# Attention, router and two feed-forward blocks on one core: even and odd heads given one layout of V, and the exponentials of the attention moved one step earlier on ScalarE

## The chip, the core and the metric

The kernel runs on one core of one Trainium2 chip. The core has TensorE (PE in the rows, with its weight loads as PEld), VectorE (DVE), ScalarE (ACT), GpSimd (POOL) and SyncE (SP, which only issues DMAs here). Each of them works through its own list of instructions in order; they meet through semaphores. PSUM is the memory that TensorE writes its results to, SBUF the working memory, and 16 DMA engines move data between SBUF and HBM. The metric is the time of one execution on the device in microseconds (us).

## What is computed

The inputs are q, k and v of 4 batches, 8 heads, 768 positions and 64 dimensions, and the weights of a router and of two feed-forward blocks. In short:

```python
scores = q @ k.T / 8                     # per batch and head, 768 x 768
keep = (key < 4) | (0 <= query - key < 128)
a = softmax(where(keep, scores, -1e9))
x = (a @ v), heads side by side          # 3072 rows x 512
logits = x @ w_gate + modality_bias[modality_id]
e = argmax(logits); p = softmax(logits)[e]
x2 = p * (relu(x @ w1[e]) @ w2[e])       # 8 experts
h = x2 @ w_in
out = (h * sigmoid(1.702 * h)) @ w_out
```

A query thus sees the first 4 positions (the sinks) and the last 128. Everything is float32. Many products are made from values that are split in a rounded and a remaining part.

## The kernel before

The attention comes first and takes about the first fifth of the time; the router, the experts and the last block follow it. The change touches the attention alone.

**Tiles and steps.** A head's 768 queries are 6 tiles of 128. A batch has 8 heads x 6 tiles = 48 tiles, and tile n of a batch is tile i = n mod 6 of head h = n div 6. All engines walk through the same numbered steps (`each_step`), and in step n each does its part for tiles of different age:

- TensorE: `scores` of tile n (L610, L611), in every second head a piece of `weigh_gates` in the head's second and third step (L667, L671), `turn_probs` of tile n-3 (transposes, L622, and for a head's last tile the sinks too, L626), and `weigh_values` of tile n-4 (L647, for the last tile of a head also L652).
- VectorE: `mask_scores` of tile n (L1090: adds the mask and takes the row's maximum, in two instructions), `move_gates` in one step of each pair of heads, `move_probs` for a head's last tile only (L1101, L1102), and in a head's fifth step `finish_head` of the head before (L1107 to L1116: row sums, reciprocals, scaled results). At the end of a batch it also sums the router's logits (L1152).
- ScalarE: `move_probs` of tile n-3 for the other five tiles of a head (L879, transposed probabilities from PSUM to SBUF), then `exps` of tile n-1 (L854), then, in the first step of a head, `pack_sinks` of the head before (L860), and `spread_sinks` once in each pair of heads (L869).
- GpSimd: `split_qk`, which splits q and k of a head in two parts, up to four heads ahead (L531 to L540).
- SyncE: the loads of q and k (L336), of V (L341 and, for the four sink rows, L343), of V transposed (L352), the stores of finished pairs of heads (L364), and pieces of w_in (L359).

**What waits for what.** Within an engine the order is the order written in its `step`. `exps` of a tile waits for that tile's mask, `turn_probs` of a tile for its `exps`, `move_probs` for the transposes, and `weigh_values` for `move_probs`. Where the steps of two batches meet, `each_step` does the new batch's step first.

**The layout of V.** Each pair of heads has for each block of keys one row of 146 words in `v_sb`: 73 for the even head and 73 for the odd one. A head's 73 are its 64 values, a one (its product is the row's sum of probabilities) and 8 router logits of the key. The even head has the order logits, one, values, the odd head values, one, logits, so that the values of both are 128 neighbouring words, which one DMA row of 512 bytes fills. `OWN`, `DEN` and `LOG` give where values, one and logits lie in each. `v_sinks` has the same layout for the four sink keys. Where the ones go, and the logits, VectorE writes with one instruction for each half of a pair.

Of the kernel before, what the change touches and what calls it, by code (L numbers as in the profile page):

```python
# [22 lines left out]
P = 128  # L23
# [4 lines left out]
ALU = mybir.AluOpType  # L28
# [12 lines left out]
def program(nc, qkT, vT, vP, modality, w_gate, bias, w1, w2, w_in, w_out, out, n_sink, window):  # L41
    B, H, D, _, S = qkT.shape
    DM = H * D
    E, _, F = w1.shape
# [40 lines left out]
    LW, VW = 64, 80  # L85
    VEXT = D + 1 + E
    OWN, DEN, LOG = (E + 1, 0), (E, D), (0, D + 1)
    VPAIR = 2 * VEXT
    COPIES = P // SINKS
# [28 lines left out]
    with ExitStack() as ctx:  # L118
# [52 lines left out]
        k_lo = place("k_lo", [P, SLOT, KEYS], F32R)  # L171
        v_sb = place("v_sb", [P, PAIRS, QT, VPAIR])
        x_sb = place("x_sb", [P, QT, DM])
# [10 lines left out]
        p_sinks = place("p_sinks", [P, P])  # L184
        v_sinks = place("v_sinks", [P, PAIRS, SINK_T, VPAIR])
        scratch = place("scratch", [P, 8])
# [144 lines left out]
        def _(sp):  # L331
# [6 lines left out]
            def load_v(b, c):  # L338

                both = slice(OWN[0], OWN[0] + P)  # L340
                sp.dma_start(v_sb[:, c, :, both], vP[b, c]).then_inc(v_loaded[c], 16)  # L341
                for t in range(SINK_T):
                    sp.dma_start(v_sinks[t * SINKS:(t + 1) * SINKS, c, t, both],  # L343
                                 vP[b, c, 0:SINKS, 0])\
                      .then_inc(v_loaded[c], 16)
# [247 lines left out]
        def _(pe):  # L593
# [35 lines left out]
            def weigh_values(b, n):  # L629
                h, i = divmod(n, QT)  # L630
                c, half = divmod(h, 2)
                if dve_takes[i]:
                    pe.wait_ge(pT_moved_dve, b * moved(True, HT) + (moved(True, n + 1) + AHEAD))
                else:
                    pe.wait_ge(pT_moved_act, b * moved(False, HT) + (moved(False, n + 1) + AHEAD))
                if i == 0:

                    pe.wait_ge(heads_done, b * H + (h - 1 + AHEAD))
                    if half == 0:
                        pe.wait_ge(v_loaded[c], b * (LOADS_V * 16) + LOADS_V * 16)  # L640
                        pe.wait_ge(vw_moved, 2 * (b * PAIRS + c + 1))
                        pe.wait_ge(sinks_marked, 2 * PAIRS + 2)
                keys = [max(i - 1, 0) + k for k in range(blocks[i])]

                o = psum[:, O_ps[h % 2], i * VW:i * VW + VEXT]
                for k, kb in enumerate(keys):
                    mm = pe.matmul(o, pT[:, n % 2, k * P:(k + 1) * P],  # L647
                                   v_sb[:, c, kb, half * VEXT:(half + 1) * VEXT],
                                   start=(i == 0 and k == 0), stop=(k == len(keys) - 1), skip_group_check=True)
                if i == QT - 1 and SINK_T:  # L650

                    mm = pe.matmul(psum[:, O_ps[h % 2], FIRST_S * VW:QT * VW]  # L652
                                   .rearrange("p (t n) -> p t n", n=VW)[:, :, 0:VEXT], pT_sinks[:],
                                   v_sinks[:, c, :, half * VEXT:(half + 1) * VEXT],
                                   start=False, stop=True, skip_group_check=True)
                mm.then_inc(pv_done, 1)

            def weigh_gates(b, c, part):

                g = b * PAIRS + c  # L660
                if part == 0:
                    pe.wait_ge(wg_loaded, 32)
                    pe.wait_ge(vt_loaded[g % 2], g // 2 * 16 + 16)
                    if g:
                        pe.wait_ge(vw_moved, 2 * g)
                for t in range(part * HALF_T, (part + 1) * HALF_T):
# [172 lines left out]
        def _(act):  # L839
# [169 lines left out]
        def _(dve):  # L1009
# [12 lines left out]
            dve.memset(wg_sb[:], 0.0).then_inc(cleared, 1)  # L1022
            for half in range(2):
                at = half * VEXT + DEN[half]
                dve.memset(v_sb[:, :, :, at:at + 1].rearrange("p c t o -> p (c t) o"), 1.0).then_inc(sinks_marked, 1)
            for s in (logits_out, xsT_split, y_moved, x2T_split, o_moved_dve):
# [77 lines left out]
            def finish_head(b, h):  # L1104
                dve.wait_ge(pv_done, b * HT + ((h + 1) * QT + AHEAD))
                heads = psum[:, O_ps[h % 2], 0:QT * VW].rearrange("p (t d) -> p t d", t=QT)
                dve.tensor_scalar(rden[:, 0, :], heads[:, :, DEN[h % 2]], 1e-9, None, ALU.add).then_inc(dve_step, 1)  # L1107
# [4 lines left out]
                dve.tensor_tensor(lg_parts[:, h, :].rearrange("p (t e) -> p t e", t=QT), heads[:, :, LOG[h % 2]:LOG[h % 2] + E],  # L1112
                                  per_row.broadcast_to([P, QT, E]), ALU.mult).then_inc(part_added, 1)
                if h % 2 == 0:
                    dve.wait_ge(x_stored[h // 2], b * 16 + DMA)
                dve.tensor_tensor(x_sb[:, :, h * D:(h + 1) * D], heads[:, :, OWN[h % 2]:OWN[h % 2] + D],  # L1116
                                  per_row.broadcast_to([P, QT, D]), ALU.mult).then_inc(heads_done, 1)

            def move_gates(b, c):
# [5 lines left out]
                for half in range(2):  # L1125
                    at = half * VEXT + LOG[half]
                    dve.tensor_tensor(v_sinks[0:rows, c, :, at:at + E],
                                      row[:, :, half * E:(half + 1) * E].broadcast_to([rows, SINK_T, E]),
                                      sink_pick[0:rows].rearrange("p (t o) -> p t o", o=1)
                                      .broadcast_to([rows, SINK_T, E]),  # L1130
                                      ALU.mult)
                for half in range(2):
                    at = half * VEXT + LOG[half]
# [279 lines left out]
```

## Time and profile before

| | |
|---|---|
| median of 3 runs | 1169.98 us (1169.49 to 1170.28) |
| the profiled execution, its own time | 1169.98 us |
| its span, first to last instruction | 1167.9 us |
| mean granted TensorE clock | 0.970 of full speed |
| TensorE busy (matmuls) | 1108.2 us, 95% |
| TensorE weight loads | 937.1 us, 80% |
| VectorE, ScalarE, GpSimd busy | 427.7, 376.6, 273.2 us |

TensorE is busy nearly everywhere. The chain that ended last, which is followed back from the last instruction through what released each step, consists of TensorE's work to 93%. A change elsewhere moves the end only where it makes TensorE wait, or ends a wait of TensorE. A matmul's end is modelled in this profile, so a short wait is seen better in the row of the weight load than in that of the matmul.

### The profile page before, as it was taken

The page shows a single profiled execution, that of the slowest core. Times are in us where ns is not written, and L with a number is a line of the kernel's source. Part 1 is how long each engine was busy: PE and PEld are TensorE (multiplying, and loading weights), DVE is VectorE, ACT ScalarE, POOL GpSimd, SP SyncE. Part 2 cuts the span into 40 slices and gives each one's busy share as a digit, 9 for nine tenths or more (in the row PEclk, how much of TensorE's full clock was granted, in tenths as well). Part 3 has the DMA queues.
Part 4 walks back from the last instruction along what each step waited for, and adds up shares of the span by engine and source line. Part 5 has one row for each costly group of instructions (what it writes and reads, how often), then busy time and mean ns, then how long its engine had stood idle before and what let it go on. Part 6 is the DMA issues. An engine that isn't in the chain of part 4 may idle for free.

```text
span 1167.9 us, 18474 instructions
## 1 busy us (share of the span) xinstructions
PE 1108.2 (95%) x5844; PEld 937.1 (80%) x5845; DVE 427.7 (37%) x1098; ACT 376.6 (32%) x779; POOL 273.2 (23%) x327
## 2 busy tenths in 40 slices
PE   9999999925999999999959999999999999999998
PEld 9999999824888888888847888888888888888886
DVE  5665666684222233212335223223322322222222
ACT  3666666512222133222325222222222222222221
POOL 8898888002751112112110000000000000000000
PEclk9999999956999999999988999999999999999999
DMA  9999997145111124111051002002001000100000
GB/s 218 244 256 233 232 229 190 47 154 184 45 44 37 45 79 150 40 45 45 27 190 54 1 1 72 0 0 72 0 0 56 16 0 27 45 0 0 36 1 36
DMA packets 58669, 91.98 MB, mean 79 GB/s; under 512 B 7936, under 2 KB 32768, under 8 KB 58624
## 3 DMA queue, kind: packets, MB, share of 16 engines
q1 hardware_dynamic: 54464, 77.79, 24.2%
q0 software_dynamic: 4160, 13.63, 3.5%
q8 instruction: 23, 0.38, 0.1%
q14 instruction: 22, 0.18, 0.1%
HBM read 72.01 MB, written 19.40 MB: 78 GB/s over the span
## 4 chain that ended last, share of the span: by engine, by line
PE 93%; DVE 3%; issue 1%; DMA 1%; ACT 1%; DVEq 0%; ACTq 0%; POOLq 0%; POOL 0%; SPq 0%
PE psum L799 8%; PE psum L800 8%; PE psum L801 8%; PE psum L816 8%; PE psum L817 8%; PE psum L818 7%; PE psum L647 6%; PE psum L731 4%; PE psum L733 4%; PE psum L732 4%; PE psum L756 4%; PE psum L758 4%; PE psum L757 4%; PE psum L622 3%; PE psum L610 2%; PE psum L743 2%
## 5 line engine op out<-in xcount | busy, mean ns | idle before, releaser
L1357 DVE TENSOR_TENSOR g<-psum,g 128x512 f32<-128x512 f32 x96 | 66.4, 691 | 312.0 <-ACT g L978 312.0
L978 ACT ACTIVATE g<-psum 128x512 f32<-128x512 f32 x96 | 57.3, 597 | 320.2 <-PE psum L801 320.1
L799 PE MATMUL psum<-x2T,win_hi 128*128 (+1 forms) x384 | 152.9, 398 | 1.4 <-DVE x2T L1349 1.4
L800 PE MATMUL psum<-x2T,win_hi 128*128 (+1 forms) x384 | 152.4, 397 | 0.0
L816 PE MATMUL psum<-w_hi,gT_hi 128*128 128x512 f32 x384 | 152.4, 397 | 0.0
L801 PE MATMUL psum<-x2T,win_lo 128*128 (+1 forms) x384 | 152.3, 397 | 0.0
L817 PE MATMUL psum<-w_lo,gT_hi 128*128 128x512 f32 x384 | 150.4, 392 | 0.0
L818 PE MATMUL psum<-w_hi,gT_lo 128*128 128x512 f32 x384 | 149.7, 390 | 0.0
L647 PE MATMUL psum<-v_sb,pT 128*128 128x73 f32 x704 | 105.9, 269 | 1.8 <-DVE pT L1102 0.3
L1090 DVE CUSTOM_DVE_ANT_0 s_msk<-psum,mask_sb 128x260 f32<-128x260 f32 (+1 forms) x192 | 74.9, 404 | 74.8 <-PE psum L611 39.7
L647 PEld LDWEIGHTS psum<-v_sb,pT 128*128 128x128 f32 x704 | 93.4, 191 | 8.3 <-DVE pT L1102 5.6
L854 ACT ACTIVATE probs<-s_msk,negmax 128x260 f32<-128x260 f32 (+1 forms) x192 | 93.4, 495 | 12.4 <-DVE negmax L1090 12.2
L1360 DVE TENSOR_TENSOR gT_lo<-g,gT_hi 128x512 fp32r<-128x512 f32 x96 | 66.5, 692 | 65.9 <-ACT gT_hi L982 65.9
L756 PE MATMUL psum<-w_hi,hT_hi 128*128 128x512 f32 x208 | 83.9, 403 | 5.8 <-DVE w_lo L1288 5.8
L799 PEld LDWEIGHTS psum<-x2T,win_hi 128*128 128x128 f32 x384 | 72.4, 189 | 18.8 <-DVE x2T L1349 1.8
L731 PE MATMUL psum<-w_hi,xsT_hi 128*128 128x512 f32 x208 | 84.6, 407 | 2.3 <-DVE xsT_lo L1303 2.3
L801 PEld LDWEIGHTS psum<-x2T,win_lo 128*128 128x128 f32 x384 | 72.4, 189 | 17.8
L800 PEld LDWEIGHTS psum<-x2T,win_hi 128*128 128x128 f32 x384 | 72.6, 189 | 16.9
L818 PEld LDWEIGHTS psum<-w_hi,gT_lo 128*128 128x128 f32 x384 | 72.1, 188 | 16.3
L816 PEld LDWEIGHTS psum<-w_hi,gT_hi 128*128 128x128 f32 x384 | 72.1, 188 | 15.8
L817 PEld LDWEIGHTS psum<-w_lo,gT_hi 128*128 128x128 f32 x384 | 72.2, 188 | 15.2
L982 ACT CAST gT_hi<-g 128x512 fp32r<-128x512 f32 x96 | 59.5, 620 | 75.6 <-DVE g L1357 75.6
(184 smaller groups left out, 1863.1 us busy)
## 6 DMA issues: line engine op xcount, KB each, us to landing
qk_raw<-qkT SPq DMA_DIRECT2D x64, 384.0 KB, 7.8
stage<-w SPq DMA_DIRECT2D x12, 1024.0 KB, 6.5
vT_sb<-vT SPq DMA_DIRECT2D x16, 384.0 KB, 7.4
v_sb<-vP SPq DMA_DIRECT2D x16, 384.0 KB
x_rows<-x_sb SPq DMA_DIRECT2D x16, 384.0 KB, 3.4
x<-y_rows SPq DMA_DIRECT2D x24, 256.0 KB, 3.2
out<-o_out SPq DMA_DIRECT2D x24, 256.0 KB, 2.1
win_raw<-w_in SPq DMA_DIRECT2D x16, 256.0 KB, 8.6
```

Of the source, the lines that this page charges most:

```text
L647: mm = pe.matmul(o, pT[:, n % 2, k * P:(k + 1) * P], v_sb[:, c, kb, half * VEXT:(half + 1) * VEXT], start=(i == 0 and k == 0), stop=(k == ...
L731: pe.matmul(psum[:, HB[hf], :], xsT_hi[:, c, :], hi, start=(c == 0), stop=False)
L756: pe.matmul(psum[:, YB, :], hT_hi[:, f, :], hi, start=(f == 0), stop=False)
L799: pe.matmul(bank, wh, hi, start=(c == 0), stop=False)
L800: pe.matmul(bank, wh, lo, start=False, stop=False)
L801: mm = pe.matmul(bank, win_lo[:, c, f * P:(f + 1) * P], hi, start=False, stop=(c == CH - 1))
L816: pe.matmul(psum[:, OB[t], :], gh, hi, start=(f == 0), stop=False)
L817: pe.matmul(psum[:, OB[t], :], gh, lo, start=False, stop=False)
L818: mm = pe.matmul(psum[:, OB[t], :], gT_lo[:, f % 4, t * P:(t + 1) * P], hi, start=False, stop=(f == F2C - 1))
L854: act.activation(probs[:, n % RING, 0:width[i]], s_msk[:, n % RING, 0:width[i]], ACT.Exp, bias=negmax[:, n % 8:n % 8 + 1], scale=-1.0).the ...
L1090: dve.tensor_tensor_reduce(s_msk[:, n % RING, 0:width[i]], psum[:, S_ps[n % 3], 0:width[i]], mask_sb[:, min(i, MASKS - 1), 0:width[i]], -S ...
L1360: dve.tensor_tensor(gT_lo[:, f % 4, :], g32[:, f % 2, :], gT_hi[:, f % 4, :].bitcast(F32), ALU.subtract).then_inc(gT_split, 1)
```

## The change

It has two parts.

**One layout for both heads of a pair.** `v_sb` and `v_sinks` get for each head a row of 80 words: 64 values, the one, 8 logits and 7 unused. The two constants `DEN`, `LOG` are the same for both heads, and `OWN` is gone. The load of V now writes 64 neighbouring words (256 bytes) at a time where it wrote 128. VectorE fills the ones and the logits of both halves with one instruction; `vw_moved` and `sinks_marked` are counted accordingly.

**ScalarE's order.** In step n it does `exps` of tile n, no longer of tile n-1, and `pack_sinks` stands ahead of it.

```diff
-    VEXT = D + 1 + E
-    OWN, DEN, LOG = (E + 1, 0), (E, D), (0, D + 1)
-    VPAIR = 2 * VEXT
+    DEN, LOG, VEXT = D, D + 1, D + 1 + E
...
-        v_sb = place("v_sb", [P, PAIRS, QT, VPAIR])
+        v_sb = place("v_sb", [P, PAIRS, QT, 2, VW])
...
-                both = slice(OWN[0], OWN[0] + P)
-                sp.dma_start(v_sb[:, c, :, both], vP[b, c]).then_inc(v_loaded[c], 16)
+                sp.dma_start(v_sb[:, c, :, :, 0:D].rearrange("p t h d -> p (t h) d"),
+                             vP[b, c].rearrange("p t h d -> p (t h) d")).then_inc(v_loaded[c], 16)
                 for t in range(SINK_T):
-                    sp.dma_start(v_sinks[t * SINKS:(t + 1) * SINKS, c, t, both],
+                    sp.dma_start(v_sinks[t * SINKS:(t + 1) * SINKS, c, t, :, 0:D],
                                  vP[b, c, 0:SINKS, 0])\
...
-                                   v_sb[:, c, kb, half * VEXT:(half + 1) * VEXT],
+                                   v_sb[:, c, kb, half, 0:VEXT],
...
             def step(b, n):
                 if TURN_LAG <= n < HT + TURN_LAG:
                     move_probs(b, n - TURN_LAG)
-                if 1 <= n <= HT:
-                    exps(b, n - 1)
                 if n % QT == 0 and n and n <= HT and SINK_T:
                     pack_sinks(b, n // QT - 1)
+                if n < HT:
+                    exps(b, n)
                 if n < HT and n % (2 * QT) == VW_AT:
                     spread_sinks(b, n // (2 * QT))
...
             for c in range(PAIRS):
-                for half in range(2):
-                    dve.tensor_copy(v_sinks[:, c, :, half * VEXT + DEN[half]], sink_pick[:]).then_inc(sinks_marked, 1)
+                dve.tensor_copy(v_sinks[:, c, :, :, DEN],
+                                sink_pick[:].rearrange("p (t o) -> p t o", o=1).broadcast_to([P, SINK_T, 2]))\
+                   .then_inc(sinks_marked, 1)
...
-                for half in range(2):
-                    at = half * VEXT + LOG[half]
-                    dve.tensor_copy(v_sb[:, c, :, at:at + E],
-                                    psum[:, VW_ps, 0:QT * LW].rearrange("p (t n) -> p t n", n=LW)
-                                    [:, :, half * E:(half + 1) * E]).then_inc(vw_moved, 1)
+                dve.tensor_copy(v_sb[:, c, :, :, LOG:VEXT],
+                                psum[:, VW_ps, 0:QT * LW].rearrange("p (t n) -> p t n", n=LW)[:, :, 0:2 * E]
+                                .rearrange("p t (h e) -> p t h e", h=2)).then_inc(vw_moved, 1)
```

How ScalarE's order moves is seen best where one head ends and the next begins. These are its instructions before, in the first batch from tile 15 of head 2 on. An exponential has `probs` as its result, a move has `pT`, packing has `p_sinks`; the shape 128x128 marks a head's first tile. In order they are: exponential 15, move 14, exponential 16, move 15, exponential 17, packing, move 16, exponentials 18 and 19, move 18.

```order
L854 ACTIVATE probs<-s_msk,negmax 128x260
L879 COPY pT<-psum 128x256
L854 ACTIVATE probs<-s_msk,negmax 128x260
L879 COPY pT<-psum 128x256
L854 ACTIVATE probs<-s_msk,negmax 128x260
L860 COPY p_sinks<-probs 128x16
L879 COPY pT<-psum 128x256
L854 ACTIVATE probs<-s_msk,negmax 128x128
L854 ACTIVATE probs<-s_msk,negmax 128x260
L879 COPY pT<-psum 128x128
```

Now ScalarE has the same stretch as follows (the lines have moved up by two). In order: exponential 16, move 14, exponential 17, move 15, packing, exponential 18, move 16, exponentials 19 and 20, move 18.

```order
L852 ACTIVATE probs<-s_msk,negmax 128x260
L877 COPY pT<-psum 128x256
L852 ACTIVATE probs<-s_msk,negmax 128x260
L877 COPY pT<-psum 128x256
L858 COPY p_sinks<-probs 128x16
L852 ACTIVATE probs<-s_msk,negmax 128x128
L877 COPY pT<-psum 128x256
L852 ACTIVATE probs<-s_msk,negmax 128x260 x2
L877 COPY pT<-psum 128x128
```

Moves and packing keep their order among themselves; each exponential has moved ahead of one move. Exponential 17 now stands ahead of move 15, where it stood behind it.

## Rows read from the trace of the kernel before

**Rows 1.** Busy time by stage: us, busy by engine (instructions), PEclk, DMA share, GB/s.
```profile
80.00:200.00 120.00, 118.98 (x979) 112.87 (x979) 73.06 (x357) 75.81 (x222) 102.86 (x110) 1.00 0.93 230
```
**Rows 2.** Waits, 0 to 230 us: who waited for whom, us, times, longest us.
```profile
DVE s_msk L1090 <- ACT probs L854: 34.4, 54, 1.1
PEld psum L647 <- DVE pT L1102: 5.4, 17, 0.5
```
**Rows 3.** Timeline: start, us, engine, line, instruction; batch 2, steps 17 to 19, heads 2 and 3.
```profile
140.46 0.51 ACT L854 ACTIVATE probs<-s_msk,negmax 128x260 f32<-128x260 f32 x1
140.52 0.16 DVE L1107 TENSOR_SCALAR rden<-psum 128x6 f32<-128x6 f32 x1
140.88 0.37 ACT L879 COPY pT<-psum 128x256 f32<-128x256 f32 x1
141.53 0.42 DVE L1090 CUSTOM_DVE_ANT_0 s_msk<-psum,mask_sb 128x260 f32<-128x260 f32 x1
141.79 0.37 ACT L879 COPY pT<-psum 128x256 f32<-128x256 f32 x1
141.88 0.08 DVE L1090 DVE_READ_ACCUMULATOR2_ANT negmax<- 128x1 f32 x1
142.39 0.53 PEld L647 LDWEIGHTS psum<-v_sb,pT 128*128 128x128 f32 x4
```
**Rows 4.** Timeline, where head 1 of batch 2 ends and head 2 begins.
```profile
134.52 0.08 DVE L1090 DVE_READ_ACCUMULATOR2_ANT negmax<- 128x1 f32 x1
135.64 0.53 PEld L647 LDWEIGHTS psum<-v_sb,pT 128*128 128x128 f32 x4
...
142.98 0.80 ACT L854 ACTIVATE probs<-s_msk,negmax 128x128 f32<-128x128 f32 x2
```
**Rows 5.** Timeline, batch 2, steps 5 to 8, behind the logits' sum of batch 1.
```profile
128.90 0.52 PEld L647 LDWEIGHTS psum<-v_sb,pT 128*128 128x128 f32 x4
129.13 0.09 DVE L1090 DVE_READ_ACCUMULATOR2_ANT negmax<- 128x1 f32 x1
129.26 0.51 ACT L854 ACTIVATE probs<-s_msk,negmax 128x260 f32<-128x260 f32 x1 [0.58 <-DVE negmax L1090]
129.82 0.20 PEld L622 LDWEIGHTS psum<-ident,probs 128*128 128x128 f32 x2 [0.17 <-ACT probs L854]
```
**Rows 6.** Timeline, the last steps of the attention.
```profile
228.96 0.52 PEld L647 LDWEIGHTS psum<-v_sb,pT 128*128 128x128 f32 x4
228.97 0.51 ACT L854 ACTIVATE probs<-s_msk,negmax 128x260 f32<-128x260 f32 x1
```
**Rows 7.** Timeline: scores of batch 2's tile 19 and the mask behind them.
```profile
142.16 0.28 PE L611 MATMUL psum<-k_lo,q_st 128*128 128x260 f32 x1
142.66 0.43 DVE L1090 CUSTOM_DVE_ANT_0 s_msk<-psum,mask_sb 128x260 f32<-128x260 f32 x1 [0.49 <-ACT probs L854]
```
**Rows 8.** DMA queue: packets, MB, share of 16 engines; 102.6 to 103.6, then 29.0 to 30.5 us.
```profile
q1 hardware_dynamic: 489, 0.28, 104.1%
...
q1 hardware_dynamic: 2759, 0.04, 107.4%
```
**Rows 9.** Timeline: GpSimd's split of head 5 of batch 0, and the head's first scores.
```profile
36.82 0.82 POOL L531 CAST q_st<-qk_raw 128x768 fp32r<-128x768 f32 x1 [2.78 <-DMA qk_raw<-qkT]
42.32 0.23 POOL L540 TENSOR_TENSOR k_lo<-qk_raw,k_hi 128x24 fp32r<-128x24 f32 x1
...
46.62 0.31 PE L610 MATMUL psum<-k_hi,q_st 128*128 128x128 f32 x1
```
**Rows 10.** Waits of SyncE, 0 to 230 us.
```profile
SPq L364 <- DVE x_sb L1116: 86.9, 14, 11.7
```
**Rows 11.** Small instructions of VectorE, and TensorE's first transposes: timeline, then groups by line.
```profile
10.39 1.96 DVE L1058 COPY v_sinks<-sink_pick 128x4 f32<-128x4 f32 x8 [0.32 <-issue]
17.02 0.14 PEld L622 LDWEIGHTS psum<-ident,probs 128*128 128x128 f32 x1
...
L1134 DVE COPY v_sb<-psum 128x48 f32<-128x48 f32 x28 | 4.4, 199 | 0.0
```

More of the change, by code:

```diff
@@ L184, in program @@
         p_sinks = place("p_sinks", [P, P])
-        v_sinks = place("v_sinks", [P, PAIRS, SINK_T, VPAIR])
+        v_sinks = place("v_sinks", [P, PAIRS, SINK_T, 2, VW])
         scratch = place("scratch", [P, 8])
@@ L640, in weigh_values @@
                         pe.wait_ge(v_loaded[c], b * (LOADS_V * 16) + LOADS_V * 16)
-                        pe.wait_ge(vw_moved, 2 * (b * PAIRS + c + 1))
-                        pe.wait_ge(sinks_marked, 2 * PAIRS + 2)
+                        pe.wait_ge(vw_moved, b * PAIRS + c + 1)
+                        pe.wait_ge(sinks_marked, PAIRS + 1)
                 keys = [max(i - 1, 0) + k for k in range(blocks[i])]
@@ L653, in weigh_values @@
                                    .rearrange("p (t n) -> p t n", n=VW)[:, :, 0:VEXT], pT_sinks[:],
-                                   v_sinks[:, c, :, half * VEXT:(half + 1) * VEXT],
+                                   v_sinks[:, c, :, half, 0:VEXT],
                                    start=False, stop=True, skip_group_check=True)
@@ L664, in weigh_gates @@
                     if g:
-                        pe.wait_ge(vw_moved, 2 * g)
+                        pe.wait_ge(vw_moved, g)
                 for t in range(part * HALF_T, (part + 1) * HALF_T):
@@ L1022, in _ @@
             dve.memset(wg_sb[:], 0.0).then_inc(cleared, 1)
-            for half in range(2):
-                at = half * VEXT + DEN[half]
-                dve.memset(v_sb[:, :, :, at:at + 1].rearrange("p c t o -> p (c t) o"), 1.0).then_inc(sinks_marked, 1)
+            dve.memset(v_sb[:, :, :, :, DEN:DEN + 1].rearrange("p c t h o -> p (c t h) o"), 1.0).then_inc(sinks_marked, 1)
             for s in (logits_out, xsT_split, y_moved, x2T_split, o_moved_dve):
@@ L1106, in finish_head @@
                 heads = psum[:, O_ps[h % 2], 0:QT * VW].rearrange("p (t d) -> p t d", t=QT)
-                dve.tensor_scalar(rden[:, 0, :], heads[:, :, DEN[h % 2]], 1e-9, None, ALU.add).then_inc(dve_step, 1)
+                dve.tensor_scalar(rden[:, 0, :], heads[:, :, DEN], 1e-9, None, ALU.add).then_inc(dve_step, 1)
                 dve.wait_ge(dve_step, b * 2 * H + 2 * h + 1)
@@ L1111, in finish_head @@
                 per_row = rden[:, 1, :].rearrange("p (t o) -> p t o", o=1)
-                dve.tensor_tensor(lg_parts[:, h, :].rearrange("p (t e) -> p t e", t=QT), heads[:, :, LOG[h % 2]:LOG[h % 2] + E],
+                dve.tensor_tensor(lg_parts[:, h, :].rearrange("p (t e) -> p t e", t=QT), heads[:, :, LOG:VEXT],
                                   per_row.broadcast_to([P, QT, E]), ALU.mult).then_inc(part_added, 1)
@@ L1115, in finish_head @@
                     dve.wait_ge(x_stored[h // 2], b * 16 + DMA)
-                dve.tensor_tensor(x_sb[:, :, h * D:(h + 1) * D], heads[:, :, OWN[h % 2]:OWN[h % 2] + D],
+                dve.tensor_tensor(x_sb[:, :, h * D:(h + 1) * D], heads[:, :, 0:D],
                                   per_row.broadcast_to([P, QT, D]), ALU.mult).then_inc(heads_done, 1)
@@ L1125, in move_gates @@
                 for half in range(2):
-                    at = half * VEXT + LOG[half]
-                    dve.tensor_tensor(v_sinks[0:rows, c, :, at:at + E],
+                    dve.tensor_tensor(v_sinks[0:rows, c, :, half, LOG:VEXT],
                                       row[:, :, half * E:(half + 1) * E].broadcast_to([rows, SINK_T, E]),
@@ L1131, in move_gates @@
                                       ALU.mult)
-                for half in range(2):
-                    at = half * VEXT + LOG[half]
-                    dve.tensor_copy(v_sb[:, c, :, at:at + E],
-                                    psum[:, VW_ps, 0:QT * LW].rearrange("p (t n) -> p t n", n=LW)
-                                    [:, :, half * E:(half + 1) * E]).then_inc(vw_moved, 1)
+                dve.tensor_copy(v_sb[:, c, :, :, LOG:VEXT],
+                                psum[:, VW_ps, 0:QT * LW].rearrange("p (t n) -> p t n", n=LW)[:, :, 0:2 * E]
+                                .rearrange("p t (h e) -> p t h e", h=2)).then_inc(vw_moved, 1)
             def step(b, n):
```

## The prediction

> **What bounds the kernel now.** I read the busy times by stage first. In the middle of the attention TensorE's matmuls fill 118.98 of 120 us and its weight loads 112.87, at a granted clock of 1.00 [rows 1]. So the attention takes what TensorE takes, plus what TensorE waits. Next come the waits. TensorE's largest one is for VectorE's move of a head's last tile, 5.4 us in 17 places [rows 2]; there is hardly another. ScalarE is busy for 75.81 of the 120 us and VectorE for 73.06 [rows 1], so neither is a bound by its sum. What matters is when each of their results is late. That is read from the timeline, where one head passes into the next, since VectorE has its longest job there. In step 17 it starts `finish_head` at 140.52, behind mask 16, and is free for mask 17 at 141.53: 1.01 us in which no mask is made [rows 3]. The mask of a head's last tile is late in every head, and the question is who stands behind it.
>
> **ScalarE's order, away from batch ends.** Before, in step 18, ScalarE does move 15 first (141.79, 0.37 us) and exponential 17 behind it. The late mask, whose maximum is there at 141.88 + 0.08 = 141.96, holds nobody up. Tile 15 is in SBUF at 142.16, and TensorE loads it at 142.39, 0.23 us later, for work it is free to do then [rows 3].
>
> After, exponential 17 stands ahead of move 15. It can't start before the mask's maximum. Rows 5 show 0.04 us between the maximum (129.13 + 0.09 = 129.22) and the exponential (129.26), so it starts at 142.00. From an exponential's start to that of the move behind it I take 0.42 us, as from 140.46 to 140.88 [rows 3], though it takes 0.51: ScalarE overlaps the ends. So move 15 starts at 142.42 and ends at 142.79. I add 0.05 us for TensorE to see it, about what a semaphore took above, and TensorE loads at 142.84 in place of 142.39. It stands still for 0.45 us. TensorE is in order: scores 20 and all that follows stand behind this load, the wait isn't made up for, and VectorE and ScalarE are driven by TensorE's scores, so they shift with it. Bounds for one wait: 0.30 if the overlap is larger than that one row shows, 0.55 if there is none.
>
> This holds where an even head ends and an odd one begins. Where an odd head ends, TensorE has a piece of `weigh_gates` in front of the same load. There the maximum is out at 134.60 and the load comes only at 135.64, 1.04 us later; exponential (0.04 + 0.42), move (0.37) and 0.05 fit in 0.88 [rows 4]. No wait. The even heads with a `finish_head` in them and no batch end are heads 2, 4 and 6 in 4 batches: 12 x 0.45 = 5.4 us (3.6 to 6.6).
>
> **At batch ends.** In the first head of batches 1 to 3, VectorE has also the sum of the logits behind `finish_head`. The maximum of tile 5 comes at 129.22, the exponential starts at 129.26 already now (ScalarE waited 0.58 us for it), and now move 3 is behind it: 129.26 + 0.42 + 0.37 + 0.05 = 130.10, and TensorE loaded tile 3 at 128.90 [rows 5]. That is 1.20 us, less 0.17 us which TensorE today waits for the same exponential a bit later (the load at 129.82) and then no longer does: 1.03 us, 3 times, 3.1 us (2.4 to 3.6).
>
> Where two batches meet, `each_step` does the new batch's step first, so that in the first step exponential 0 of the new batch too is ahead of move 45. By the same kind of place [rows 4]: 134.60 + 0.04 + 0.42, a 128-wide exponential at 0.80 - 0.51 = 0.29, then 0.37 and 0.05, is 135.77 against 135.64. That is 0.13 us, 3 times, 0.4 us (0 to 0.8).
>
> At the attention's end no scores stand between the steps. Exponential 47 starts at 228.97 and is now ahead of move 45: 228.97 + 0.42 + 0.37 + 0.05 = 229.81 against TensorE's load at 228.96 [rows 6]. That is 0.85 us (0.4 to 0.9), and the router waits for this end.
>
> **What an earlier exponential gives.** Exponentials are ready one turn sooner for the transposes. TensorE's waits for them are the 0.17 us counted above. The larger wait, for VectorE's move of the last tile, stays: it hangs on mask 20 and the transposes, which follow TensorE's scores.
>
> **The layout.** TensorE's instructions keep their count and shapes. VectorE does 4 small copies fewer at the start, of the 8 that take 1.96 us, about 1 us less ahead of its first mask; but TensorE's own list reaches the first transposes at 17.02, 4.7 us after those copies end (10.39 + 1.96 = 12.35) [rows 11], so nothing comes of it. The copy of logits comes once for a pair instead of twice, at 199 ns each [rows 11], 16 x 0.2 = 3.2 us of VectorE in all if none of it is lost to the longer copy. It lies in a pair's fourth step, where VectorE has no `finish_head`, so it is worth nothing here. The larger clearing of `v_sinks` at the start lies ahead of VectorE's first wait for q and k. I cost these at 0, between -1 and 0.
>
> The load of V goes from 768 packets of 512 bytes to 1536 of 256: on each of 16 engines 96 packets instead of 48. The trace has no packet of 256 bytes. Nearly all packets of the one window are of 512 bytes: 16 x 1.0 us x 1.041 / 489 = 34 ns each. Those of the other are nearly all of 8 bytes: 16 x 1.5 x 1.074 / 2759 = 9.3 ns [rows 8]. A packet of 256 bytes lies between these ends, by a straight line at 22 ns. One load of V then takes 2.1 us of each engine instead of 1.6, +0.5 us (-0.7 to +1.6). Is it hidden? The DMA engines are 0.93 busy [rows 1], 12.5 us of each 13.49, the time of a pair of heads (the same load of a fourth tile stands at 128.90 and one pair later at 142.39 [rows 3, 5]). With 0.5 us more they still keep up. The tightest place is early: the q and k of head 5 land at 36.8 behind four loads of V, GpSimd waited 2.78 us for them, is done at 42.55, and TensorE takes them at 46.62, 4.07 us later [rows 9]. Four loads cost 2.0 us (-2.8 to +6.4), so it is hidden, up to 2.3 us at the upper end. SyncE waits 86.9 us for finished heads [rows 10], so a longer issue of these DMAs has room. I cost the layout at 0, between -1 and +2.3.
>
> A rule that speaks against this: the Trainium skill, DMA: Bandwidth & Descriptors, Specifications, says that below 512 bytes a DMA engine reads, modifies and writes. Packets of 8 bytes at 9.3 ns [rows 8] don't look like it, and no row here shows 256. By that rule the sum would be that of the third rival.
>
> **The sum.** 5.4 + 3.1 + 0.4 + 0.85 + 0 = 9.7 us. The profiled execution took 1169.98 us (span 1167.9, 2.1 around it), equal to the median: 1179.7 us. With the bounds of each term, 6.4 to 11.9 without the layout, and up to 1.5 us more for waits of some hundredths that I may have missed, the forecast's own range is 1176.4 to 1183.4.
>
> **The rivals.**
> 1. Faster. The waits name ScalarE's exponential as what VectorE's masks wait for, 34.4 us in 54 places [rows 2]. If a mask did wait for the exponential just ahead, an earlier exponential would bring the mask of a head's third tile sooner, and with it the move of the last tile, for which TensorE waits 5.4 us [rows 2]. It decides if the mask follows ScalarE: then -5.4 us, 1164.6. Against it: the mask at 142.66 comes 0.22 us after the scores' end (142.16 + 0.28 = 142.44) [rows 7], and by the code a mask needs the exponential of six tiles before. 6%.
> 2. No change: ScalarE's delay is absorbed, because TensorE's load at 142.39 isn't the first thing that needs move 15, or the late mask comes sooner in the new layout. It needs 0.45 us of slack that I don't see: between the move's end and the load lie 0.23 us [rows 3], and these are counted. 1170. 8%.
> 3. DMA. If a packet of 256 bytes costs a whole 512-byte packet twice, 68 ns, a load of V takes 6.5 us, +4.9. Four of them make the q and k of head 5 19.6 us later, against 4.07 of slack: 15.5 us of standstill. A pair's DMA work is then 12.5 + 4.9 = 17.4 us against 13.49, 3.9 us for each of the 12 later pairs, 47 us: about 1233. For it speaks the nearly full DMA share, against it the price of the 8-byte packets. 4%.
>
> **How the numbers follow.** The forecast has 82%. This kernel's runs lie within 0.07%, and I take 0.2% (2.3 us) as what can be told from no change. Slower by more: 82 + 4 = 86%; within: 8%; faster: 6%. The range is the forecast's own, taken down to 1175.0 for waits that are partly given back, and up to 1184.5 for the bound of the DMA.
>
> **What would show it.** ScalarE's idle time for VectorE's maximum should grow from a few places to about one a head. TensorE's weight load for L647 should have new waits of about 0.45 us, released by ScalarE's move, in every second head, and 1.2 us at three batch starts; the attention should end about 10 us later, with the stages behind it unchanged. GpSimd should wait a little longer for q and k of head 5, TensorE not at all. The prediction is wrong if the attention ends within 2 us of before, or if the new waits are on q and k.

## The result, and the profile after

| | before | after |
|---|---|---|
| time, median (lowest to highest) of 4 runs, us | 1169.8 (1169.49 to 1170.28) | 1180.42 (1180.31 to 1182.43) |
| profiled execution, us (its span) | 1169.98 (1167.9) | 1180.94 (1178.2) |
| TensorE's first scores of the last head, us | 221.97 | 231.19 |
| router's first matmul, us | 236.76 | 247.08 |

The changed kernel takes 1.0095 times as long (95% interval 1.0077 to 1.0112). It is slower, and the predicted 1179.7 us is 0.7 us off. The attention ends 10.32 us later and the span is 10.3 us longer, so all of it is in the attention. How the sum came about is another matter: both parts of the change can cost something, and one of them I had put at nothing.

From the page of the kernel after: its span, and the busy time, share and instructions of each engine.

```profile
span 1178.2 us, 18453 instructions
PE 1111.5 (94%) x5844; PEld 937.2 (80%) x5845; DVE 425.7 (36%) x1077; ACT 381.0 (32%) x779; POOL 273.5 (23%) x327
DMA packets 71213, 91.98 MB, mean 78 GB/s; under 512 B 33024, under 2 KB 45312, under 8 KB 71168
```

Its middle of the attention, in the columns of [rows 1]:

```profile
80.00:200.00 120.00, 116.18 (x943) 108.67 (x943) 68.93 (x332) 74.94 (x212) 99.46 (x107) 1.00 0.98 229
```

TensorE executes the same 5844 matmuls, but in the same 120 us 943 where there were 979, at the same clock. It is not slower, it stands still. The waits of the kernel after, 0 to 245 us (who waited for whom, us, times, longest), say for whom:

```profile
ACT probs L852 <- DVE negmax L1087: 50.8, 82, 9.3
DVE s_msk L1087 <- ACT probs L852: 40.5, 53, 1.5
...
PEld psum L645 <- ACT pT L877: 9.0, 17, 1.1
PEld psum L645 <- DVE pT L1099: 7.8, 25, 0.6
...
PEld psum L669 <- ACT vT_sinks L867: 0.9, 1, 0.9
```

The row for ScalarE's move of `pT` is the largest of TensorE's and is new: [rows 2] has only VectorE's, and that one has grown too. One place of each kind, in the timeline of after. First the place of [rows 3], the end of head 2 of batch 2:

```profile
146.75 0.08 DVE L1087 DVE_READ_ACCUMULATOR2_ANT negmax<- 128x1 f32 x1
146.87 0.52 ACT L852 ACTIVATE probs<-s_msk,negmax 128x260 f32<-128x260 f32 x1 [0.58 <-DVE negmax L1087]
147.29 0.35 ACT L877 COPY pT<-psum 128x256 f32<-128x256 f32 x1
...
147.69 0.52 PEld L645 LDWEIGHTS psum<-v_sb,pT 128*128 128x128 f32 x4 [0.39 <-ACT pT L877]
```

The maximum is out at 146.83, the exponential starts at 146.87, the move 0.42 us after it, the load 0.40 us after that. These are the steps of the prediction, each within 0.05 us. Then the place of [rows 5], behind the logits' sum:

```profile
131.80 0.82 DVE L1146 TENSOR_REDUCE lg<-lg_parts 128x48 f32<-128x384 f32 x1
133.00 0.51 ACT L852 ACTIVATE probs<-s_msk,negmax 128x260 f32<-128x260 f32 x1 [1.32 <-DVE negmax L1087]
133.42 0.35 ACT L877 COPY pT<-psum 128x256 f32<-128x256 f32 x1
133.82 0.52 PEld L645 LDWEIGHTS psum<-v_sb,pT 128*128 128x128 f32 x4 [1.14 <-ACT pT L877]
```

The attention's end, to be held against [rows 6]:

```profile
238.61 0.51 ACT L852 ACTIVATE probs<-s_msk,negmax 128x260 f32<-128x260 f32 x1 [0.58 <-DVE negmax L1087]
239.03 0.35 ACT L877 COPY pT<-psum 128x256 f32<-128x256 f32 x1
239.43 0.52 PEld L645 LDWEIGHTS psum<-v_sb,pT 128*128 128x128 f32 x4 [0.70 <-ACT pT L877]
```

And one that the prediction does not have, behind `pick_biases` in step 36 of the last batch:

```profile
223.88 0.17 DVE L1072 CAST mod_f<-mod_i 128x24 f32<-128x24 int32 x1
...
225.30 0.36 DVE L1078 TENSOR_TENSOR bias_of<-bias_of,r_a 128x192 f32<-128x192 f32 x1
225.88 0.43 DVE L1087 CUSTOM_DVE_ANT_0 s_msk<-psum,mask_sb 128x260 f32<-128x260 f32 x1 [0.22 <-PE psum L609]
226.35 0.51 ACT L852 ACTIVATE probs<-s_msk,negmax 128x260 f32<-128x260 f32 x1 [0.86 <-DVE negmax L1087]
226.77 0.28 ACT L867 COPY vT_sinks<-vT_sb 128x128 f32<-128x128 f32 x1
227.10 0.30 PEld L669 LDWEIGHTS psum<-wg_sb,vT_sinks 128*128 128x128 f32 x2 [0.86 <-ACT vT_sinks L867]
```

VectorE picks the biases from 223.88 to 225.66, so mask 37 is late. Its exponential stands in the new order ahead of `spread_sinks` too (ScalarE's copy that writes `vT_sinks`), and `weigh_gates` needs that one's result.

To count all places, I take the first scores of every head in both timelines and look at how much further apart they are at each than at the one before. Heads are counted 0 to 31, and "head 4" here is the stretch from its first scores to those of head 5.

| growth ahead of | times | each, us | predicted |
|---|---|---|---|
| heads 4, 6, 8, 12, 14, 20, 22, 24, 28, 30 (and 16: 0.26) | 11 | 0.40 to 0.43 | 0.45 |
| heads 10, 18, 26 | 3 | 1.13, 1.14, 1.20 | 1.03 |
| heads 9, 17, 25 | 3 | 0.09, 0.08, 0.09 | 0.13 |
| head 2 | 1 | 0.23 | 0 |
| head 31 | 1 | 0.94 | 0 |
| router (last even head, and the end) | 1 | 1.10 | 0.45 + 0.85 |
| all others | | -0.04 to 0.01 | 0 |

At head 2 TensorE waits for VectorE's move of the last tile of head 0, 0.60 us where it waited 0.35. What makes that move late there was not followed up.

The DMA side of the profile had a surprise that did not show in this time. SyncE's issues of the first loads (start, us, engine), first of the kernel before:

```profile
6.32 1.57 SPq L343 DMA_DIRECT2D v_sinks<-vP  x4
...
31.00 0.58 SPq L352 DMA_DIRECT2D vT_sb<-vT  x1
```

and of the kernel after:

```profile
6.33 5.71 SPq L341 DMA_DIRECT2D v_sinks<-vP  x4
...
34.72 0.58 SPq L350 DMA_DIRECT2D vT_sb<-vT  x1
```

The same four small DMAs, issued behind a load of V in 256-byte packets, hold SyncE for 5.71 us instead of 1.57. The three later groups of four took 3.26, 5.23 and 4.27 us before and take 4.93, 5.94 and 1.76 after, so that the four groups together hold it for 18.3 us instead of 14.3. The load of the third pair's transposed V is issued 3.7 us later and lands at 40.7 (34.72 + 6.0, the time to landing of that issue) instead of 38.4 (31.00 + 7.4). TensorE's `weigh_gates` took it at 40.33 before and takes it at 40.92 after. So 1.9 us of slack have become 0.2. It is hidden in this execution only because TensorE is already 0.6 us later there (0.40 us for the new order, 0.23 at head 2).

### The profile page after: what moved, and what is told of

Read it like the earlier page. It is cut to its first block, busy times and chain, and to the rows that moved or that the text cites. A ratio compares the mean times of both kernels' runs of the same rounds, so it can differ in the third digit from the quotient of the medians.

```text
span 1178.2 us, 18453 instructions
## 1 busy us (share of the span) xinstructions
PE 1111.5 (94%) x5844; PEld 937.2 (80%) x5845; DVE 425.7 (36%) x1077; ACT 381.0 (32%) x779; POOL 273.5 (23%) x327
## 4 chain that ended last, share of the span: by engine, by line
PE 91%; DVE 3%; ACT 2%; issue 2%; DMA 1%; DVEq 0%; ACTq 0%; POOLq 0%; POOL 0%; SPq 0%
PE psum L797 8%; PE psum L798 8%; PE psum L799 8%; PE psum L814 8%; PE psum L815 7%; PE psum L816 7%; PE psum L645 6%; PE psum L729 4%; PE psum L731 4%; PE psum L730 4%; PE psum L754 4%; PE psum L756 4%; PE psum L755 4%; PE psum L620 3%; PE psum L608 2%; PE psum L741 2%
## 5 line engine op out<-in xcount | busy, mean ns | idle before, releaser
L852 ACT ACTIVATE probs<-s_msk,negmax 128x260 f32<-128x260 f32 (+1 forms) x192 | 94.6, 494 | 68.2 <-DVE negmax L1087 50.8
```

What stands on the lines that cost most here:

```text
L852: act.activation(probs[:, n % RING, 0:width[i]], s_msk[:, n % RING, 0:width[i]], ACT.Exp, bias=negmax[:, n % 8:n % 8 + 1], scale=-1.0).the ...
```

## The experiments

Every comparison is the median against that of the kernel before in the same series. Per-head growths are read as in the table above. The expectations were written against 1169.98 us, while the kernel before took 1170.48 us (the runs e), 1171.29 (f) and 1170.6 (g and h) in its three series; so e1, f2 and f4 lie 0.2 to 0.3 us above the ranges expected for them, and within them by their ratios.

**The two parts alone.** The kernel before with only ScalarE's new order:

```diff
-                if 1 <= n <= HT:
-                    exps(b, n - 1)
                 if n % QT == 0 and n and n <= HT and SINK_T:
                     pack_sinks(b, n // QT - 1)
+                if n < HT:
+                    exps(b, n)
```

> The kernel before with ScalarE's new order alone, the layout of V as before. My theory (exponentials stand ahead of moves while the mask of a head's last tile is late): the whole loss, 1180.0 us (1179.3 to 1180.8), TensorE's loads for L647 with 0.40 us of wait for ScalarE's move in every second head and 1.1 us at three batch starts. Rival (the layout's smaller DMA packets or wider rows share in the loss): 1172 to 1178.

Measured: 1181.14 us, ratio 1.009 (1.0077 to 1.0103). Its growths are those of the kernel after: 0.41 to 0.43 at the even heads, 1.14, 1.14 and 1.16, 0.93 at head 31, 1.11 at the end. Its waits:

```profile
PEld psum L647 <- ACT pT L879: 9.1, 17, 1.2
PEld psum L647 <- DVE pT L1102: 6.9, 21, 0.5
```

The order alone makes the whole difference. Only the 0.23 at head 2 is not there, and head 16 has the full 0.42 where after has 0.26; e2, below, has +0.24 and -0.16 at these two, so they are the layout's, and nearly cancel.

The complement, the changed kernel with the old order (the same lines turned round):

> The changed kernel with ScalarE's old order: the layout of V alone. My theory: 1169.6 us (1169.0 to 1170.4), within the noise of before, although a load of V has twice the packets; GpSimd waits some us more for q and k of head 5 and TensorE nothing. Rival (DMA or layout costs): 1172 or more.

Measured: 1177.21 us, ratio 1.0054 (1.0041 to 1.0067). A miss by 7.6 us. Beside the 0.24 at head 2 (and the -0.16 at head 16) it has a single growth, 7.54 us in head 4. The weight load there, and the stretches around it (us, busy by engine, clock, DMA share, GB/s):

```profile
42.81 1.28 PEld L665 LDWEIGHTS psum<-wg_sb,vT_sb 128*128 128x128 f32 x6 [2.87 <-issue]
```
```profile
42.00:44.00 2.00, 1.15 (x6) 1.19 (x7) 0.00 (x0) 0.00 (x0) 1.92 (x4) 0.73 1.03 230
44.00:46.00 2.00, 2.00 (x12) 2.00 (x11) 0.00 (x0) 1.25 (x4) 1.92 (x2) 0.50 0.96 215
...
54.00:56.00 2.00, 2.00 (x20) 2.00 (x19) 0.75 (x6) 1.89 (x7) 1.92 (x3) 1.00 1.03 221
```

"issue" hides a DMA here: transposed V is issued at 35.83 and lands 6.9 us later, at 42.73. TensorE stands still for 2.87 us, and then its granted clock is 0.50, the 1.2 GHz level, until about 53. A wait of 2.9 us thus costs 7.5.

**Is it the small packets?** The kernel before, with its V loaded by two DMAs of 256-byte packets instead of one of 512:

```diff
-                sp.dma_start(v_sb[:, c, :, both], vP[b, c]).then_inc(v_loaded[c], 16)
+                for half in range(2):
+                    one = slice(OWN[0] + half * D, OWN[0] + half * D + D)
+                    sp.dma_start(v_sb[:, c, :, one], vP[b, c, :, :, half]).then_inc(v_loaded[c], 16)
```

> The kernel before, its layout kept, but V is loaded by two DMAs of 64 words a row instead of one of 128: packets of 256 bytes as in the new layout, and one more DMA to issue for each pair. Theory (the size and number of packets make the loads behind them late): a standstill at head 4, 1174 to 1179 us. Rival (the wider rows or VectorE's merged instructions are at fault): 1170 to 1171.

Measured: 1177.42 us, ratio 1.0059 (1.0046 to 1.0073). The profiled execution took 1180.26 us and grows by 9.41 us in head 4 and nowhere else. The same standstill, without the new layout of SBUF:

```profile
44.84 1.36 PEld L669 LDWEIGHTS psum<-wg_sb,vT_sb 128*128 128x128 f32 x6 [4.41 <-issue]
```

SyncE is held by the first `v_sinks` for 4.99 us here as well. The packet size (with one more DMA to issue for each pair) is the cause.

**And is the late load all of it?** The layout alone, with the third pair's transposed V issued ahead of the loads of V for pairs 2 to 4:

```diff
             load_qk(0, SLOT)
+            load_vt(2)
             for c in range(1, PAIRS):
...
-                if h == SLOT + 1:
-                    load_vt(2)
```

> The layout alone, with the load of V transposed of the third pair put ahead of the loads of V for pairs 2 to 4 instead of behind them. Theory (all that the layout costs is TensorE's standstill at head 4 for this load, with the clock that falls behind it): 1170.3 us (1169.5 to 1171.5). Rival (the layout's smaller packets cost in other places too): 1173 or more.

Measured: 1171.66 us, ratio 1.0005 (0.9996 to 1.0014): no difference from before; by the ratios 5.7 us of the layout's loss are gone. What is left, in the timeline, is the place that the prediction had called the tightest, at about a seventh of that price:

```profile
41.62 0.82 POOL L528 CAST q_st<-qk_raw 128x768 fp32r<-128x768 f32 x1 [6.24 <-DMA qk_raw<-qkT]
...
47.38 0.19 PEld L607 LDWEIGHTS psum<-k_hi,q_st 128*128 128x128 f32 x1 [1.13 <-POOL k_lo L537]
```

The 4.07 us of slack [rows 9] are used up there too, once this load stands ahead in the queue.

The changed kernel, once more as it is, in the same series:

> The changed kernel itself, once more beside the kernel before. In its profile TensorE did not stand still at head 4 for V transposed of the third pair (it landed 34.72 + 6.0 = 40.7, about when it was needed), while the layout alone stood still there. Theory: the changed kernel is at the edge of that wait, 1180 to 1183 us, with single runs some us apart. Rival (the layout's cost is there in every run and the two parts overlap otherwise): 1180.4 again in every run.

Measured: 1182.31 us, ratio 1.0094 (1.0078 to 1.0109). Its profiled execution has the late load that the first one just missed, and the clock in the stretch behind it stayed up:

```profile
42.00 0.74 PEld L665 LDWEIGHTS psum<-wg_sb,vT_sb 128*128 128x128 f32 x6 [1.21 <-issue]
```
```profile
44.00:46.00 2.00, 2.00 (x19) 1.85 (x18) 1.18 (x5) 0.82 (x3) 1.92 (x2) 1.00 1.04 227
```

In the changed kernel's two executions the load thus landed at 40.7 and 42.0 us (35.17 + 6.8), in e2 at 42.7.

And the changed kernel with the transposed V early, by the edit above:

> The changed kernel with the same earlier load of V transposed. Theory: no standstill at head 4 in any run, only the waits behind the late masks, 1180.0 us (1179.3 to 1180.8), its runs close together. Rival (the standstill is never there in the changed kernel): the same as the changed kernel beside it, to 0.3 us.

Measured: 1181.11 us, ratio 1.0085 (1.0071 to 1.0099), 1.2 us below its neighbour f1, with intervals that overlap. The wait for the late load is gone; TensorE waits 0.33 us for q and k of head 5 instead, and the even head behind it, which grew by 0.42, grows by 0.03. In the changed kernel the layout therefore costs 0 to 1.3 us, where alone it costs 7: the parts are not additive. In part TensorE's own lateness covers the load: it was ready for it at 39.94 us in e2 (42.81 less 2.87) and at 40.8 and 40.9 in the changed kernel's two executions. The rest is that the load landed 0.8 and 2.0 us sooner there, for which no run shows the reason, and that the clock did not fall behind the shorter wait.

**Taking the exponential away again.** The changed kernel, with the exponential of a head's last tile held back behind the next step's move (and at a batch's start exponential 0 behind packing):

```diff
+                if n and n % QT == 0 and n <= HT:
+                    exps(b, n - 1)
                 if n % QT == 0 and n and n <= HT and SINK_T:
                     pack_sinks(b, n // QT - 1)
-                if n < HT:
+                if n < HT and n % QT != QT - 1 and not (b and n == 0):
                     exps(b, n)
+                if n == HT and b < B - 1:
+                    exps(b + 1, 0)
```

> The changed kernel, but the exponential of a head's last tile (5 of 6 keep the early place) is held back one step, behind the move, as before. My theory, that only the late mask of a last tile matters: the waits of 0.40 and 1.13 us go, all but about 1 us of the 10.6 come back, 1170.0 to 1171.5. Rival (any early exponential delays the moves a little, in all tiles): 1174 to 1178.

Measured: 1180.05 us, but from 1173.4 to 1181.07, ratio 1.0073 (1.0054 to 1.0092). By the time alone this would have refuted the theory. The heads say otherwise: the eleven growths of 0.42 are gone, and the three of 1.13 are down to 0.29, 0.30 and 0.21. But with them went the cover of the late load. The load in the timeline, and a stretch behind it:

```profile
42.12 0.74 PEld L665 LDWEIGHTS psum<-wg_sb,vT_sb 128*128 128x128 f32 x6 [1.93 <-issue]
```
```profile
44.00:46.00 2.00, 2.00 (x13) 2.00 (x12) 0.56 (x3) 0.29 (x3) 1.92 (x2) 0.53 1.04 234
```

4.99 us at one head, with the clock down again. The scatter between runs fits a load that sometimes comes early enough. So it was run with the transposed V early as well:

> The changed kernel with V transposed of the third pair loaded earlier, and the exponential of a head's last tile held back behind the move as before; the other five tiles of a head keep the early place. Theory, with the standstill at head 4 out of the way: 1173.2 us (1172.2 to 1174.2), no wait of 0.40 us behind a late mask, about 0.3 us left at batch starts, 0.9 us at head 30 where VectorE also makes the router's biases, and about 1 us for q and k of head 5. Rival (an early exponential costs in other tiles too): 1176 or more.

Measured: 1175.14 us, ratio 1.004 (1.0026 to 1.0053), 0.9 us above the expected bound. By the ratios that is 5.3 us less than the changed kernel with the same early load. The order's waits are gone but for 0.2 to 0.3 us at the batch starts (and 0.94 at the biases, as expected); in their place TensorE waits for q and k of head 5. Its wait, and then the stretches behind it:

```profile
PEld psum L607 <- POOL k_lo L537: 1.6, 1, 1.6
```
```profile
48.00:50.00 2.00, 2.00 (x17) 2.00 (x18) 0.74 (x4) 1.35 (x5) 1.92 (x4) 0.88 1.12 362
50.00:52.00 2.00, 2.00 (x11) 2.00 (x11) 1.06 (x4) 1.12 (x3) 1.92 (x2) 0.50 1.10 234
```

That is 1.69 us and, with the lower clock, 1.23 more: 2.9 in all, which the expectation had too small.

**Making the mask early instead.** If the wait comes from the mask being behind `finish_head`, then it should also go when ScalarE keeps its new order and VectorE makes the mask first:

```diff
             def step(b, n):
-                if n < HT:
+                if n < HT and n % QT != QT - 1:
                     mask_scores(b, n)
+                if n < HT and n % QT == QT - 2:
+                    mask_scores(b, n + 1)
```

> The changed kernel, ScalarE's new order kept, but VectorE makes the mask of a head's last tile ahead of finish_head instead of behind it. My theory, that the loss is the wait behind this mask: the 0.40 us waits go and the batch starts lose part (there the next mask is late instead), 1172.5 us (1171.5 to 1174.0). Rival (the order itself costs ScalarE or TensorE, whoever delays the mask): 1178 or more.

Measured: 1173.86 us, ratio 1.0035 (1.0023 to 1.0047). Right. The waits at the even heads are gone, and the list of waits has now:

```profile
PEld psum L645 <- DVE pT L1099: 5.6, 16, 0.6
...
PEld psum L645 <- ACT pT L877: 2.5, 7, 0.5
...
PEld psum L669 <- ACT vT_sinks L867: 1.2, 1, 1.2
```

TensorE's waits for VectorE are back at 5.6 us (5.4 in [rows 2], to 230 us), and of the 9.0 us for ScalarE's move 2.5 remain. The growths left are 1.07 at the late load, 0.28 to 0.45 at each batch's start (over its first two heads), 0.24 at head 2 and 1.26 at the biases. The late load and the biases with their own remedies, the transposed V early and the biases a step later:

```diff
-                if b == B - 1 and n == HT - 2 * QT:
+                if b == B - 1 and n == HT - 2 * QT + VW_AT:
                     pick_biases()
```

> The changed kernel with ScalarE's new order kept, V transposed loaded earlier, the mask of a head's last tile made ahead of finish_head, and the router's biases made one step later, behind the mask of the head's second tile. Theory (each of the waits is VectorE's lateness before an exponential that stands ahead of a move): 1173.0 us (1171.8 to 1174.0), and the 0.9 us at head 30 gone. Rival (the order itself costs): 1176 or more.

Measured: 1172.95 us, ratio 1.0017 (1.0008 to 1.0026), as expected. The growth at head 31 falls from 1.26 to 0.18, while that of the late load has become one of 0.75 for q and k of head 5. The first shows the term that the prediction lacked to be that of the biases.

**A longer `finish_head`.** The changed kernel with the transposed V early, and one more copy in `finish_head`, into a buffer that nobody reads:

```diff
+                dve.tensor_copy(spare[:], ones[:])
```

> The changed kernel with V transposed loaded earlier and finish_head longer by one more copy of 128x128, about 0.2 us. Theory: the late mask is later by as much, and with it the move: the waits in even heads grow from 0.40 to 0.60 us, those at batch starts from 1.13 to 1.33, odd heads begin to wait by some hundredths: +4.3 us over the same kernel without the copy (1181.1), 1185.4 (1184.0 to 1187.5). Rival (the waits are not VectorE's lateness): within 1 us of 1181.1.

Measured: 1195.74 us, ratio 1.0214 (1.02 to 1.0228), 10 us more than expected (the profiled execution took 1199.9). The copy was three times as long as I had taken it (its group by line: busy us, mean ns), and the waits grew with it:

```profile
L1111 DVE COPY spare<-ones 128x128 f32<-128x128 f32 x29 | 19.6, 677 | 0.0
```
```profile
PEld psum L645 <- ACT pT L877: 22.5, 28, 1.7
```

The response itself follows the theory. From batch 1 on the copy takes 0.63 us in nearly all heads, 0.56 from its start to the next instruction's; the even heads' growth goes from 0.42 to 0.96, 0.54 more. The odd heads, which had 0.16 us of slack (1.04 less 0.88 in the prediction), now grow by 0.35. At the starts of batches 2 and 3 it is 2.8 to 2.9, and there the clock drops again, as one such start and the stretch behind it show:

```profile
143.87 0.67 PEld L645 LDWEIGHTS psum<-v_sb,pT 128*128 128x128 f32 x4 [1.66 <-ACT pT L877]
```
```profile
144.00:146.00 2.00, 2.00 (x11) 2.00 (x12) 0.49 (x3) 0.90 (x3) 1.92 (x2) 0.55 0.91 247
```

In batch 0 the growths are uneven, up to 1.75 us, because the copy is: it takes 0.22 to 1.75 us. The trace shows what its length goes by. In all 27 places where GpSimd was busy as it started, it ended 0.08 or 0.09 us after the end of the GpSimd instruction beside it; in the 5 places where GpSimd was idle it took 0.22 us. One of the long ones, the wait that it led to, and the stretch behind that, where the clock stayed up:

```profile
48.84 1.82 POOL L533 TENSOR_TENSOR q_st<-qk_raw,q_st 64x768 fp32r<-64x768 f32 x1
49.33 1.42 DVE L1111 COPY spare<-ones 128x128 f32<-128x128 f32 x1
...
52.41 0.52 PEld L645 LDWEIGHTS psum<-v_sb,pT 128*128 128x128 f32 x4 [1.72 <-ACT pT L877]
```
```profile
52.00:54.00 2.00, 1.59 (x14) 1.59 (x15) 0.53 (x5) 1.44 (x6) 2.00 (x4) 1.00 1.04 231
```

**A faster version.** The kernel before waits for VectorE's move of a head's last tile [rows 2]. At odd heads VectorE can do it ahead of the mask of the third tile, which has room. Old layout, old order, transposed V early:

```diff
+                first = n < HT and n % (2 * QT) == QT + 2
+                if first:
+                    move_probs(b, n - TURN_LAG)
...
-                if TURN_LAG <= n < HT + TURN_LAG:
+                if not first and TURN_LAG <= n < HT + TURN_LAG:
```

> The kernel before, its layout and ScalarE's order kept, with two edits: in odd heads VectorE moves the last tile of the head before ahead of the mask of the third tile, not behind it, and V transposed of the third pair is loaded earlier. Theory (TensorE's wait of 0.35 us in every odd head hangs on VectorE's mask that stands ahead of this move): 0.22 us less in 16 heads, 3.5 us, 1167.8 (1166.5 to 1169.0). Rival (the mask made later delays ScalarE's exponential and a move behind it by as much): 1171 or slower.

Measured: 1168.79 us, ratio 0.9982 (0.9973 to 0.9991): slightly faster than both kernels. Its wait for that move:

```profile
PEld psum L646 <- DVE pT L1101: 2.5, 16, 0.3
```

The 5.4 us of [rows 2] are 2.5, and the growth is -0.19 to -0.22 at 11 of the even-numbered heads and at the router, -0.36 at head 16 and nothing at heads 10, 18 and 26. The router starts 3.08 us earlier, the span is 1.2 us shorter. Behind the router's start, where none of the kernels is edited, the executions differ by 0 to 1.9 us (931.1 before and after, 933.0 here), which is why tenths are read from the heads and not from the span. How much of the gain the early load has was not run apart; TensorE has no wait for it in the kernel before, and the growth of head 4, which it would change, is -0.01.

## Why the prediction was right, and where it was not

**ScalarE's order, even heads.** Right in mechanism and size: 0.42 each against 0.45, shown by the order alone (all there), by the held exponential and the early mask (both take them away), and by the longer `finish_head` (grows with it, one to one). It was not what a total of busy time can tell: ScalarE does the same work.

**Batch starts, boundaries, end.** 1.13 to 1.20 against 1.03, 0.09 against 0.13, and 1.10 for the last even head and the end against 1.30. Right in mechanism, the first forecast a tenth too low, the last a sixth too high.

**Odd heads.** No wait, as worked out. The slack of 0.16 us was real: with 0.56 more they wait 0.35, where 0.40 would be left over.

**Rival 1** had the largest number of the waits behind it, 34.4 us of masks "waiting for exponentials". It has fallen: exponentials came a turn sooner, and that row went up, from 34.4 to 40.5 us. Masks follow the scores. **Rival 2** has fallen with the first growths; the 0.23 us between move and load were no slack.

**The missed place.** +0.9 us at the biases. The prediction looked for what else makes VectorE late only at batch starts (the logits' sum); `pick_biases` is the third such job, once in the program. With the 0.23 at head 2 this makes some 1.2 us that the sum of 9.7 lacked, and the batch starts gave 0.4 more than forecast. The even heads (with the 0.16 less at head 16), the boundaries and the end fell 0.9 short of it. That the sum came out within a microsecond is in part luck.

**The layout: the step that failed.** "I cost the layout at 0, between -1 and +2.3" and "the tightest place is early: the q and k of head 5". Alone it cost 7 us. Two things were wrong. First, the queue was counted in bytes in flight and SyncE's issuing was given room from its waits later on [rows 10]; but in the first 35 us SyncE does not wait (its issues stand without a gap), it is itself the queue, and it was held in the issuing of small DMAs. Second, the place: transposed V of the third pair stands behind the same loads and had 1.9 us of slack, less than the 4.07 of q and k. The granted clock, which fell behind the wait and cost 4.7 of the 7.5 us, was in no term. Early on every load behind the long one must be held against the time its user comes, not only the one with a visible wait. In the changed kernel this came to 0 to 1.3 us, in part because the order's delay covered it, so the time came out right in spite of it. That is luck. **Rival 3** stays fallen as priced: in the 5 us from 25 to 30, nearly all in 256-byte packets, after has

```profile
q1 hardware_dynamic: 3115, 0.79, 98.8%
```

16 x 5 x 0.988 / 3115 = 25 ns a packet, against 22 assumed, 68 in the rival, and 34 for 512 bytes [rows 8]. A load of V thus costs each engine some 0.8 us more (96 packets at 25 ns against 48 at 34), not 0.5, within the bounds of that term. The rule of the Trainium skill (DMA: Bandwidth & Descriptors, Specifications) that line rate needs transfers of at least 512 bytes, and that below them the engine reads, modifies and writes, is thus borne out here in the bytes moved per second, 0.79 MB in 5 us, 158 GB/s (0.28 MB in 1.0 us, 276 GB/s, in the window of 512-byte packets of [rows 8]), and not in a packet that costs more than one of 512. Whether the engine reads before it writes, no run here shows. What was to show it went as written for TensorE's load and for the stages behind. ScalarE's waits for the maximum grew more than written, from 5 places to 82 (12.2 to 50.8 us), where about one a head was forecast; GpSimd's wait at head 5 grew from 2.78 to 4.48 us and TensorE did not wait for it.

## What to carry to other kernels

In an in-order engine the price of putting an instruction ahead of another is the wait that it brings along: for each place, write down when its input is there and when the one behind it is needed. Two parts of a change are measured apart, since a wait in one can cover a late transfer of the other, and an experiment that removes only the first may look like a refutation. A standstill of TensorE is worth a look at the granted clock behind it.

## What the runs showed of the hardware

- TensorE's granted clock and a standstill of the otherwise full engine: it stayed at 1.00 (2.4 GHz) after 1.01 (e4), 1.13 (f2), 1.14 (after), 1.21 (f1), and in h3 after 1.44 and 1.72 us; it went to 0.50 (1.2 GHz) with 1.64 (h1), 1.66 and 1.67 (h3), 1.93 (e3), 2.87 (e2) and 4.41 us (f3). The length of the standstill alone thus does not tell which it will be. The clock fell while TensorE stood still in f3, as it went on in e2, and 0.3 to 2 us later in h3, h1 and e3, and stayed low for some 3 us (h1, h3), 7 (e3), 10 (e2) and 14 us (f3). In e2 it cost 4.7 us on top of the 2.87 waited.
- SyncE is held while it issues. In batch 0 four DMAs of 2 KB took from 1.57 to 5.23 us behind a load in 512-byte packets (before), and from 1.76 to 5.94 us behind the same bytes in 256-byte ones (after); the first such group took 1.57 us in the one case and 5.0 to 5.7 us in the other (after, f1, e2 and f3).
- A VectorE copy of 128x128 fp32 from SBUF to SBUF took 0.22 us with GpSimd idle, and beside a GpSimd instruction it ended 0.08 or 0.09 us after that one's end, after 0.22 to 1.75 us (h3, 32 copies). Nothing was changed to test whether it waits for GpSimd, but the 27 ends leave little else. A copy of the same shape out of PSUM took 0.29 us in the mean (289 ns, 32 times before).
